# Causal attention in front of two feed-forward layers: the last rows of q and k are prepared beside q, and the turned tiles of a pair move one place

## The chip, the cores and the metric

One core of one Trainium2 chip runs the whole program. The metric is the device time of one execution in microseconds (us), the median of several.

## The reference

Attention runs over 4 batches of 8 heads, 576 positions of 64 elements. A query of block i (64 positions) sees the keys of the blocks up to i. The result, written as 2304 rows of 512, goes through a dense feed-forward layer (512 to 2048 to 512, ELU) and then a layer with 8 experts, of which each row uses at most one. The change touches only the attention:

```
scores = scale * np.matmul(q, k.transpose(0, 1, 3, 2))
scores = np.where(block_i >= block_j, scores, -1e9)
scores = scores - np.max(scores, axis=-1, keepdims=True)
attn = np.exp(scores)
attn = attn / (np.sum(attn, axis=-1, keepdims=True) + 1e-09)
return np.matmul(attn, v)
```

## The kernel before

Attention works on 16 pairs of heads. The two heads of a pair lie side by side on the partitions, 64 each. The 576 positions are four full tiles of 128 and one of 64, tile 4 (`LAST`), in which both heads share the 128 partitions. Every engine runs its own program, written as `step(kk, i)`, once for each pair n = 2*kk + i and twice more to drain. Steps 0 and 1 and the last four are unrolled; between them a loop holds two steps. Semaphores with counted values order the engines. Nothing is scheduled by a compiler: the order of the lines is the order of each engine's work.

In the step of pair n (`now`) five things lie side by side:

- **Scores of n.** TensorE multiplies q by k, tile after tile (`scores(n, i, u)`, L498 on), into the four banks of `s_ps`. Tiles 1 to 4 use three products of high and low halves of float32, so `scores(n, i, 0)` waits until the halves of this pair's q and k are there (`split_lo`). VectorE takes the row maximum (`row_max`, L332 and L335), ScalarE the exponential with its row sum (`exp`, L455).
- **Turning the probabilities.** TensorE transposes them through `t_ps`, a PSUM tensor of just two banks (`turn_pair` for tiles 0 and 1, `turn_head` for tiles 2 and 3, `turn_last` for tile 4, all by L533), and VectorE copies them to `pt` (L343, L351, L357, L364). The tiles 3 and 4 of pair n-1 (`past`) are turned in the step of n. The transposed reciprocals of the row sums and the last corner of tile 4 travel with tile 0 of n: `turned_corner` (L364) copies the corner and then the reciprocals to `r_rows` (L369).
- **Preparing pair n+1 (`after`).** TensorE transposes the raw q and k through the same two banks of `t_ps` (`prep`, L492): part 0 is q's four tiles, part 1 k's four tiles, part 2 the last 64 rows of both (`raw_tail`). ScalarE copies each part to `qk_f` (`prep_copy`: L436, L438, and L441 with L443). GpSimd then splits `qk_f` into halves in two pieces (`split`, L293 and L296): q's columns once part 0 is there, all the rest, k and the last rows, once all three parts are there (`prep_out` at 3n+3). After that it splits a slice of the next layer's weights (`wi_halves`, L304 and L309).
- **Values of n-1 and n-2.** TensorE multiplies v by `pt` into `o_ps` (`values`, L591), in a first part for `past` and a second part for `older` (n-2).
- **Final product of n-2.** VectorE multiplies `o_ps` by the reciprocals (`final`, L380). They have made a trip through memory for it: `r_rows` is stored (`store_recips`, L218) and loaded again, spread over the partitions, by four DMAs (`load_recips`, L224 and L227).

All DMAs are issued by SyncE, in one order per step: `load_v(n)`, `store(n-2)`, `store_recips(n-1)`, `load_qk(n+3)`, `load_recips(n-1)`, `load_wi(n+1)`. So the six DMAs of `load_qk` (up to the step of pair 12, the last that has any) stand between the store of the reciprocals and their load. `final` of a pair waits for its four loads (`r_in`), one step later.

Of the kernel before, what the change touches and what calls it, by code (L numbers as in the profile page):

```python
# [53 lines left out]
def attention(nc, q, k, v, attn_t, w_in, wi, x_raw, x_in):  # L54
# [27 lines left out]
    with ExitStack() as ctx:  # L82
# [243 lines left out]
        def _(dve):  # L326
# [11 lines left out]
            def turned_pair(n, i, u):  # L338

                wait(dve, pt_done, turns(n, u))  # L340
                c = u + 1
                bank = 1 - u
                dve.tensor_copy(pt[i][:, :, 0:c, u * P:(u + 1) * P],  # L343
                                t_ps[:, bank, 0:2 * c * P].rearrange("p (h j w) -> p h j w", h=2, w=P))\
                   .then_inc(turned, 1)
# [15 lines left out]
            def turned_corner(n, i, last):  # L361
# [3 lines left out]
                                      t_ps[0:TAIL, 1, 2 * P:3 * P].rearrange("p (h w) -> p h w", h=2))  # L365
# [3 lines left out]
                dve.tensor_copy(r_rows[:, :], t_ps[0:COLS, 1, R0:R0 + P]).then_inc(r_row_done, 1)  # L369
# [28 lines left out]
            def step(kk, i):  # L398
# [16 lines left out]
                if now:  # L415
                    turned_pair(*now, 0)
                    row_max(now[0], 3)
# [8 lines left out]
        def _(act):  # L426
            def prep_copy(n, i, g, bank):
# [9 lines left out]
                elif g == 1:  # L437
# [47 lines left out]
        def _(pe):  # L485
            def prep(n, i, g, bank):
# [3 lines left out]
                tiles = [raw[i][:, g, t] for t in range(FULL)] if g < 2 else [raw_tail[i]]  # L490
# [44 lines left out]
            def turn_pair(n, u, ahead=None, past=None):  # L535

                c = u + 1
                bank = 1 - u
                wait(pe, exp_done, exps(n, u, 1))
                if u == 0:  # L540
                    wait(pe, turned, turns(n - 1, LAST))
                    wait(pe, rec_done, n)
                elif ahead:
                    wait(pe, prep_out, 3 * ahead[0] + 2)
                else:
                    wait(pe, turned, turns(n - 1, 3, 0))
                for h in range(2):
                    for j in range(c):
                        last = turn(bank, (h * c + j) * P, prob[u][h][:, j * P:(j + 1) * P])
                if u == 0 and past:  # L550
                    turn(bank, 2 * P, prob4[:, FULL * P:S])
                    last = turn(bank, R0, recip[:, :])
                last.then_inc(pt_done, 1)

            def turn_head(n, u, h, ahead=None):

                wait(pe, exp_done, exps(n, u, h))
                if u == 3:
                    wait(pe, turned, turns(n, 2, h))
                elif h == 0:  # L560
                    wait(pe, turned, turns(n, 1))
                elif ahead:
                    wait(pe, prep_out, 3 * ahead[0] + 3)
                else:
                    wait(pe, turned, turns(n, 0))
# [11 lines left out]
            def turn_corner(n):  # L577

                wait(pe, turned, turns(n, LAST))
                wait(pe, rec_done, n + 1)  # L580
                turn(1, 2 * P, prob4[:, FULL * P:S])
                turn(1, R0, recip[:, :]).then_inc(pt_done, 1)

            def values(n, i, part):
                if part == 0:
                    wait(pe, turned, turns(n + 1, 0))
# [17 lines left out]
            def step(kk, i):  # L604
# [12 lines left out]
                if past:  # L617
                    turn_last(past[0])
                if now:
                    scores(*now, 2)  # L620
                    if after:
                        wait(pe, prep_out, 3 * after[0] + 1)
                        prep(*after, 1, 0)
                    turn_pair(now[0], 0, past=past)
                    scores(*now, 3)
                    turn_pair(now[0], 1, after)
                    if after:
                        wait(pe, turned, turns(now[0], 0))
                        prep(*after, 2, 1)
# [1195 lines left out]
```

## Time and profile before

| | |
|---|---|
| Median of 3 executions | 883.6 us (881.44 to 883.68) |
| The profiled execution | 883.7 us, of it 882.0 us span |
| TensorE busy (matmul) | 807.8 us, 92% of the span |
| VectorE, ScalarE, GpSimd busy | 538.2, 337.5, 241.4 us |
| Mean granted TensorE clock | 0.974 of full speed |
| Attention, from the first instruction to the last `final` | about 249 us |

The span is the time from the first to the last instruction of the core. "S" below is the moment at which TensorE begins the scores of a pair (L520), and "+3.4" means 3.4 us behind the S of that step. Idle time that the profile gives in brackets is that just before an instruction, with the operation that ended it.

### The profile page before, as it was taken

The page shows a single profiled execution, that of the slowest core. Times are in us where ns is not written, and L with a number is a line of the kernel's source. Part 1 is how long each engine was busy: PE and PEld are TensorE (multiplying, and loading weights), DVE is VectorE, ACT ScalarE, POOL GpSimd, SP SyncE. Part 2 cuts the span into 40 slices and gives each one's busy share as a digit, 9 for nine tenths or more (in the row PEclk, how much of TensorE's full clock was granted, in tenths as well). Part 3 has the DMA queues.
Part 4 walks back from the last instruction along what each step waited for, and adds up shares of the span by engine and source line. Part 5 has one row for each costly group of instructions (what it writes and reads, how often), then busy time and mean ns, then how long its engine had stood idle before and what let it go on. Part 6 is the DMA issues. An engine that isn't in the chain of part 4 may idle for free.

```text
span 882.0 us, 14734 instructions
## 1 busy us (share of the span) xinstructions
PE 807.8 (92%) x4618; PEld 672.2 (76%) x4619; DVE 538.2 (61%) x1318; ACT 337.5 (38%) x815; POOL 241.4 (27%) x232
## 2 busy tenths in 40 slices
PE   5787877888769999999999999999998899999995
PEld 4565655656559888888889888889886677887884
DVE  3565766666643337856866866863575699465342
ACT  3444545454323332222223223222345277354241
POOL 1545465455334411201201100210011222321221
PEclk9889999899989999999999999999999899999998
DMA  5344445453242431202002101013142389545100
GB/s 121 84 113 120 130 121 136 112 158 103 80 146 62 136 96 57 67 6 84 19 1 81 28 1 72 25 53 138 48 128 103 113 298 348 195 152 185 40 25 8
DMA packets 102913, 88.10 MB, mean 100 GB/s; under 512 B 66676, under 2 KB 78340, under 8 KB 102736
## 3 DMA queue, kind: packets, MB, share of 16 engines
q1 hardware_dynamic: 99808, 82.48, 30.2%
q0 software_dynamic: 3056, 5.00, 1.7%
q8 instruction: 26, 0.43, 0.2%
q14 instruction: 23, 0.19, 0.1%
HBM read 72.26 MB, written 18.34 MB: 103 GB/s over the span
## 4 chain that ended last, share of the span: by engine, by line
PE 66%; DVE 2%; issue 1%; DVEq 1%; ACT 0%; POOL 0%; POOLq 0%; ACTq 0%
PE h_ps L1570 11%; PE out_ps L1570 11%; PE h_ps L1571 11%; PE h_ps L1572 10%; PE out_ps L1572 10%; PE out_ps L1571 10%; PE out_ps L1705 1%; PE tr_ps L1670 1%; PE lg_ps L1621 1%; DVEq L871 0%; DVE xt_lo L1278 0%; DVE ht_lo L1317 0%; PE tr_ps L1610 0%; DVE x2t L1307 0%; DVE tile_ids L1287 0%
## 5 line engine op out<-in xcount | busy, mean ns | idle before, releaser
L1408 ACT ACTIVATE ex<-h_ps 128x384 f32<-128x384 f32 x96 | 47.2, 492 | 275.8 <-PE h_ps L1572 275.8
L1570 PE MATMUL h_ps<-xt_hi,wi_hi 128*128 128x384 f32 x384 | 132.3, 344 | 8.2 <-DVE xt_lo L1278 8.2
L1571 PE MATMUL h_ps<-xt_lo,wi_hi 128*128 128x384 f32 x384 | 130.3, 339 | 0.0
L1572 PE MATMUL h_ps<-xt_hi,wi_lo 128*128 128x384 f32 x384 | 130.3, 339 | 0.0
L1246 DVE TENSOR_SCALAR ex<-ex 128x384 f32<-128x384 f32 x96 | 35.1, 365 | 143.2 <-ACT ex L1408 142.1
L1570 PE MATMUL out_ps<-wo_hi,gt 128*128 128x512 f32 x288 | 114.6, 398 | 0.0
L1572 PE MATMUL out_ps<-wo_hi,gt 128*128 128x512 f32 x288 | 113.9, 396 | 0.0
L1571 PE MATMUL out_ps<-wo_lo,gt 128*128 128x512 f32 x288 | 113.3, 393 | 0.0
L455 ACT ACTIVATE prob<-s_ps,negmax 128x128 f32<-128x128 f32 (+2 forms) x144 | 77.7, 548 | 92.0 <-DVE negmax L332 92.0
L332 DVE TENSOR_REDUCE negmax<-s_ps 128x2 f32<-128x256 f32 (+1 forms) x64 | 51.3, 823 | 52.0 <-PE s_ps L528 49.0
L1128 DVE CUSTOM_DVE_ANT_0 x2t<-x,w_raw 128x512 bf16<-128x512 f32 x108 | 82.8, 807 | 0.4
L1570 PEld LDWEIGHTS h_ps<-xt_hi,wi_hi 128*128 128x128 f32 x384 | 72.5, 189 | 12.2 <-DVE xt_lo L1278 8.8
L1571 PEld LDWEIGHTS h_ps<-xt_lo,wi_hi 128*128 128x128 f32 x384 | 72.6, 189 | 3.1
L1572 PEld LDWEIGHTS h_ps<-xt_hi,wi_lo 128*128 128x128 f32 x384 | 72.5, 189 | 0.0
L1034 POOL DMA_INDIRECT route_table<-entry,slot x18 | 20.9, 1163 | 177.2 <-DVE slot L1207 161.0
L533 PE MATMUL t_ps<-ident,prob 128*128 128x128 f32 (+1 forms) x400 | 66.1, 300 | 2.6 <-DVE pt L357 0.9
L1026 POOL TENSOR_TENSOR xt_lo<-x_raw,xt_hi 128x384 fp32r<-128x384 f32 x20 | 28.4, 1419 | 142.6 <-ACT xt_hi L1422 142.4
L293 POOL TENSOR_TENSOR qk_hi<-qk_f,one 128x512 fp32r<-128x512 f32 (+1 forms) x30 | 36.0, 1200 | 106.2 <-ACT qk_f L436 54.5
L1572 PEld LDWEIGHTS out_ps<-wo_hi,gt 128*128 128x128 f32 x288 | 54.1, 188 | 13.4
L1570 PEld LDWEIGHTS out_ps<-wo_hi,gt 128*128 128x128 f32 x288 | 54.1, 188 | 9.4 <-DVE gt L1239 0.8
L1571 PEld LDWEIGHTS out_ps<-wo_lo,gt 128*128 128x128 f32 x288 | 54.1, 188 | 8.9
L533 PEld LDWEIGHTS t_ps<-ident,prob 128*128 128x128 f32 (+1 forms) x400 | 48.1, 151 | 12.5 <-issue 6.7
(174 smaller groups left out, 1661.7 us busy)
## 6 DMA issues: line engine op xcount, KB each, us to landing
w_raw<-in_moe_w_dram SPq DMA_DIRECT2D x56, 512.0 KB, 5.2
attn_t<-attn_sb SPq DMA_DIRECT2D x16, 288.0 KB, 2.1
x_raw<-attn_t SPq DMA_DIRECT2D x24, 192.0 KB, 2.5
out_dram<-x SPq DMA_DIRECT2D x18, 256.0 KB, 2.1
x_rows<-x SPq DMA_DIRECT2D x18, 256.0 KB, 2.5
raw_qk<-in_q_dram SPq DMA_DIRECT2D x32, 128.0 KB, 2.3
raw_qk<-in_k_dram SPq DMA_DIRECT2D x32, 128.0 KB, 2.4
v<-in_v_dram SPq DMA_DIRECT2D x32, 128.0 KB, 2.5
```

The costliest lines, as they stand in the source:

```text
L293: pool.tensor_tensor(qk_hi[i][:, a:b], qk_f[i][:, a:b], one[:, :].to_broadcast([P, b - a]), ALU.mult).then_inc(split_hi, 1)
L332: dve.tensor_reduce(heads_cols(negmax, u), s_pair(u), AX_X, ALU.max, negate=True).then_inc(max_done, 1)
L455: act.activation(dst, src, ACT.Exp, bias=negmax[:, c:c + 1], accum_out=rowsum[i][:, c:c + 1]).then_inc(exp_done, 1)
L533: return pe.transpose(t_ps[0:src.shape[1], bank, at:at + P], src, ident[:, :])
L1026: pool.tensor_tensor(xtk(b % 2, 1, k), x_raw[k][:, :], xtk(b % 2, 0, k).bitcast(F32), ALU.subtract).then_inc(x_lo_done, 1)
L1034: pool.indirect_dma_start(table, bass.IndirectOffsetOnAxis(ap=slot[j][:, 0:1], axis=0), entry[j][:, :], None, bounds_check=E * N - 1, oob_ ...
L1128: ins = dve.tensor_tensor_reduce(dot_rows[:, ((E + 1) * t + e) % 2], x2[s][:, :], all_skip if e == E else all_gates[:, e, :], 1.0, 0.0, AL ...
L1246: dve.tensor_scalar(e, e, 1.0, -1.0, ALU.min, ALU.add).then_inc(em_done, 1)
L1408: act.activation(ex[:, f % 2], h_ps[:, f % 2, 0:NB], ACT.Exp).then_inc(ex_done, 1)
L1570: pe.matmul(dst, stat[0], mov[0], start=start, stop=False, skip_group_check=True)
L1571: pe.matmul(dst, stat[0], mov[1], start=False, stop=False, skip_group_check=True)
L1572: return pe.matmul(dst, stat[1], mov[0], start=False, stop=stop, skip_group_check=True)
```

## The change

Five edits, all in the attention, which belong together because the two banks of `t_ps` change hands in another order:

1. The order of the preparation becomes q, last rows, k. The last rows are now part 1: TensorE transposes them right behind q, into bank 1, and ScalarE copies them right behind q. k is part 2, in bank 0, transposed behind the scores of tile 2 and copied ahead of the exponentials of tile 2.
2. `turn_last` (tile 4 of the past pair) moves from ahead of the scores of tile 2 to behind k's transposes. It now waits for ScalarE's copy of the last rows.
3. `turn_pair` for tile 0, with the corner and the reciprocals, moves behind the scores of tile 3 and from bank 1 to bank 0; tile 1 changes to bank 1 and waits for VectorE's copy of tile 4.
4. VectorE follows: reciprocals, `final`, maximum of tile 2, copy of tile 4, maximum of tile 3, corner and `r_rows`, tile 0, tile 1, maximum of tile 4.
5. `values` of the first part waits for the copy of tile 4, of the second part for that of the next pair's tile 0.

The cut diff:

```diff
@@ def step(kk, i), VectorE
                 if past:
                     for h in range(2):
                         turned_head(*past, 3, h)
+                if past:
+                    recips(past[0])
                 if older:
                     final(*older)
+                if now:
+                    row_max(now[0], 2)
                 if past:
-                    recips(past[0])
                     turned_last(*past)
                 if now:
-                    row_max(now[0], 2)
+                    row_max(now[0], 3)
                 if past:
                     turned_corner(*past, last=not now)
                 if now:
                     turned_pair(*now, 0)
-                    row_max(now[0], 3)
                     turned_pair(*now, 1)
@@ def step(kk, i), ScalarE
                     if after:
                         prep_copy(*after, 0, 0)
-                        prep_copy(*after, 1, 0)
+                        prep_copy(*after, 1, 1)
+                        prep_copy(*after, 2, 0)
                     exp(*now, 2)
                     exp(*now, 3)
-                    if after:
-                        prep_copy(*after, 2, 1)
                     exp(*now, LAST)
@@ def prep, TensorE
-                tiles = [raw[i][:, g, t] for t in range(FULL)] if g < 2 else [raw_tail[i]]
+                tiles = [raw_tail[i]] if g == 1 else [raw[i][:, g // 2, t] for t in range(FULL)]
@@ def turn_last
-            def turn_last(n):
+            def turn_last(n, ahead):
                 wait(pe, exp_done, exps(n, LAST, 0))
-                wait(pe, turned, turns(n, 3, 1))
+                wait(pe, *((prep_out, 3 * ahead[0] + 2) if ahead else (turned, turns(n, 3, 1))))
@@ def step(kk, i), TensorE
                 if after:
                     wait(pe, turned, turns(past[0], 3, 0)) if past else pe.wait_ge(prep_out, 3)
                     prep(*after, 0, 0)
-                if past:
-                    turn_last(past[0])
+                    wait(pe, turned, turns(past[0], 3, 1)) if past else pe.wait_ge(prep_out, 3)
+                    prep(*after, 1, 1)
                 if now:
                     scores(*now, 2)
-                    if after:
-                        wait(pe, prep_out, 3 * after[0] + 1)
-                        prep(*after, 1, 0)
-                    turn_pair(now[0], 0, past=past)
+                if after:
+                    wait(pe, prep_out, 3 * after[0] + 1)
+                    prep(*after, 2, 0)
+                if past:
+                    turn_last(past[0], after)
+                if now:
                     scores(*now, 3)
-                    turn_pair(now[0], 1, after)
-                    if after:
-                        wait(pe, turned, turns(now[0], 0))
-                        prep(*after, 2, 1)
+                    turn_pair(now[0], 0, after, past)
+                    turn_pair(now[0], 1)
                     scores(*now, LAST)
```

No instruction is added or taken away on ScalarE, VectorE, GpSimd or SyncE, and no DMA changes; what moves shows in each engine's order.

ScalarE, one step (here step 0, which is unrolled): before, the first L436 and L438 are the copies of q and k, L441 and L443 those of the last rows, L455 the exponentials by width.

```order
L436 ACTIVATE qk_f<-t_ps 128x512
L438 ACTIVATE qk_f<-t_ps 128x512
L455 ACTIVATE prob_0,rowsum<-s_ps,negmax 128x384
L455 ACTIVATE prob_1,rowsum<-s_ps,negmax 128x384
L455 ACTIVATE prob_0,rowsum<-s_ps,negmax 128x512
L455 ACTIVATE prob_1,rowsum<-s_ps,negmax 128x512
L441 ACTIVATE qk_f<-t_ps 64x64 x2
L443 ACTIVATE qk_f<-t_ps 128x64
L455 ACTIVATE prob,rowsum<-s_ps,negmax 128x576
```

ScalarE, the same step after the change (the lines are numbered one higher):

```order
L437 ACTIVATE qk_f<-t_ps 128x512
L442 ACTIVATE qk_f<-t_ps 64x64 x2
L444 ACTIVATE qk_f<-t_ps 128x64
L439 ACTIVATE qk_f<-t_ps 128x512
L456 ACTIVATE prob_0,rowsum<-s_ps,negmax 128x384
L456 ACTIVATE prob_1,rowsum<-s_ps,negmax 128x384
L456 ACTIVATE prob_0,rowsum<-s_ps,negmax 128x512
L456 ACTIVATE prob_1,rowsum<-s_ps,negmax 128x512
L456 ACTIVATE prob,rowsum<-s_ps,negmax 128x576
```

The copy that completes `prep_out` is now k's, ahead of four exponentials; before it was that of the last rows, behind them.

VectorE, one step of the loop before, from `final` to the maximum of tile 4 (L335); L332 are the maxima of tiles 2 and 3, L357 is tile 4, L364 and L369 the corner and `r_rows`, L343 tiles 0 and 1:

```order
L380 TENSOR_TENSOR attn_sb<-o_ps,r_sb 128x576
...
L374 RECIPROCAL recip<-guarded 128x9
...
L357 COPY pt<-t_ps 128x4x2x64
...
L332 TENSOR_REDUCE negmax<-s_ps 128x2
...
L364 COPY pt<-t_ps 64x2x64
...
L369 COPY r_rows<-t_ps 9x128
...
L343 COPY pt<-t_ps 128x2x128
...
L332 TENSOR_REDUCE negmax<-s_ps 128x2
...
L343 COPY pt<-t_ps 128x2x2x128
...
L335 TENSOR_REDUCE negmax<-s_ps 128x1
```

VectorE, the same place after the change:

```order
L373 RECIPROCAL recip<-guarded 128x9
...
L379 TENSOR_TENSOR attn_sb<-o_ps,r_sb 128x576
...
L332 TENSOR_REDUCE negmax<-s_ps 128x2
...
L356 COPY pt<-t_ps 128x4x2x64
...
L332 TENSOR_REDUCE negmax<-s_ps 128x2
...
L363 COPY pt<-t_ps 64x2x64
...
L368 COPY r_rows<-t_ps 9x128
...
L342 COPY pt<-t_ps 128x2x128
...
L342 COPY pt<-t_ps 128x2x2x128
...
L335 TENSOR_REDUCE negmax<-s_ps 128x1
```

The copy to `r_rows` now stands behind the maximum of tile 3.

## Rows read from the trace of the kernel before

**Rows 1.** Stretches: from:to, length, each engine's busy time, granted clock, DMA share, GB/s.

```profile
55.10:71.50 16.40, 13.95 (x99) 10.31 (x99) 9.25 (x16) 6.96 (x24) 7.64 (x7) 0.81 0.43 112
86.60:167.80 81.20, 66.51 (x596) 49.51 (x596) 53.76 (x96) 41.43 (x144) 45.81 (x37) 1.00 0.48 129
```

**Rows 2.** Waits in the attention: engine, line, released by: us in total, times, longest.

```profile
PE s_ps L520 <- POOL qk_lo L296: 37.0, 15, 2.7
```

**Rows 3.** Timeline, TensorE, one step of the loop: start, us, engine, line, operation [idle before].

```profile
100.10 0.49 PE L520 MATMUL s_ps<-qk_f 64*128 64x128 f32 x4 [2.44 <-POOL qk_lo L296]
...
113.63 0.49 PE L520 MATMUL s_ps<-qk_f 64*128 64x128 f32 x4 [2.45 <-POOL qk_lo L296]
```

**Rows 4.** Timeline, ScalarE and GpSimd, the same step.

```profile
105.67 0.60 ACT L438 ACTIVATE qk_f<-t_ps 128x512 f32<-128x512 f32 x1 [1.11 <-PE t_ps L492]
105.83 1.28 POOL L296 TENSOR_TENSOR qk_lo<-qk_f,qk_hi 128x512 fp32r<-128x512 f32 x1
...
109.72 0.43 ACT L441 ACTIVATE qk_f<-t_ps 64x64 f32<-64x64 f32 x2
...
110.47 1.36 POOL L293 TENSOR_TENSOR qk_hi<-qk_f,one 128x704 fp32r<-128x704 f32 x1 [3.36 <-ACT qk_f L443]
...
111.91 1.66 POOL L296 TENSOR_TENSOR qk_lo<-qk_f,qk_hi 128x704 fp32r<-128x704 f32 x1
```

**Rows 5.** Timeline, VectorE, the same step.

```profile
103.53 0.76 DVE L380 TENSOR_TENSOR attn_sb<-o_ps,r_sb 128x576 f32<-128x576 f32 x1 [0.18 <-issue]
...
104.33 0.67 DVE L357 COPY pt<-t_ps 128x512 f32<-128x512 f32 x1
105.08 0.96 DVE L332 TENSOR_REDUCE negmax<-s_ps 128x2 f32<-128x768 f32 x1
106.10 0.28 DVE L364 COPY pt<-t_ps 64x128 f32<-64x128 f32 x1
106.31 0.27 DVE L369 COPY r_rows<-t_ps 9x128 f32<-9x128 f32 x1
...
107.05 1.23 DVE L332 TENSOR_REDUCE negmax<-s_ps 128x2 f32<-128x1024 f32 x1
```

**Rows 6.** Timeline, SyncE's DMA issues, the same step and the next.

```profile
106.64 0.31 SPq L218 DMA_DIRECT2D recip_rows<-r_rows  x1
107.91 0.97 SPq L195 DMA_DIRECT2D raw_qk<-in_q_dram  x2
...
111.83 0.50 SPq L224 DMA_DIRECT2D r_sb<-recip_rows  x1
...
118.10 0.66 SPq L197 DMA_DIRECT2D v<-in_v_dram  x1
119.22 0.37 SPq L211 DMA_DIRECT2D attn_t<-attn_sb  x1
```

**Rows 7.** Timeline, the last pair: its reciprocals are stored, loaded and used.

```profile
242.36 0.29 SPq L218 DMA_DIRECT2D recip_rows<-r_rows  x1
243.59 0.45 SPq L224 DMA_DIRECT2D r_sb<-recip_rows  x1
...
248.12 0.76 DVE L380 TENSOR_TENSOR attn_sb<-o_ps,r_sb 128x576 f32<-128x576 f32 x1 [5.78 <-issue]
```

**Rows 8.** Timeline: S of pair 1, `final` of pairs 0 and 11, S of pair 15.

```profile
26.02 0.49 PE L520 MATMUL s_ps<-qk_f 64*128 64x128 f32 x4 [2.66 <-POOL qk_lo L296]
...
45.04 0.76 DVE L380 TENSOR_TENSOR attn_sb<-o_ps,r_sb 128x576 f32<-128x576 f32 x1 [1.42 <-PE o_ps L591]
...
202.65 0.76 DVE L380 TENSOR_TENSOR attn_sb<-o_ps,r_sb 128x576 f32<-128x576 f32 x1 [0.18 <-issue]
...
226.39 0.49 PE L520 MATMUL s_ps<-qk_f 64*128 64x128 f32 x4 [2.48 <-POOL qk_lo L296]
```

**Rows 9.** DMA issues in the attention: transfer, count, KB each, median us to landing.

```profile
x_raw<-attn_t SPq DMA_DIRECT2D x4, 192.0 KB, 3.7
...
r_sb<-recip_rows SPq DMA_DIRECT2D x30, 16.0 KB, 2.5
```

More of the change, by code:

```diff
@@ L341, in turned_pair @@
                 c = u + 1
-                bank = 1 - u
                 dve.tensor_copy(pt[i][:, :, 0:c, u * P:(u + 1) * P],
-                                t_ps[:, bank, 0:2 * c * P].rearrange("p (h j w) -> p h j w", h=2, w=P))\
+                                t_ps[:, u, 0:2 * c * P].rearrange("p (h j w) -> p h j w", h=2, w=P))\
                    .then_inc(turned, 1)
@@ L364, in turned_corner @@
                 ins = dve.tensor_copy(pt[i][0:TAIL, :, FULL, FULL * P:S],
-                                      t_ps[0:TAIL, 1, 2 * P:3 * P].rearrange("p (h w) -> p h w", h=2))
+                                      t_ps[0:TAIL, 0, 2 * P:3 * P].rearrange("p (h w) -> p h w", h=2))
                 if last:
@@ L368, in turned_corner @@
                 wait(dve, r_stored, 16 * n)
-                dve.tensor_copy(r_rows[:, :], t_ps[0:COLS, 1, R0:R0 + P]).then_inc(r_row_done, 1)
+                dve.tensor_copy(r_rows[:, :], t_ps[0:COLS, 0, R0:R0 + P]).then_inc(r_row_done, 1)
             def recips(n):
@@ L436, in prep_copy @@
                     act.activation(qk_f[i][:, Q:K], src[:, :], ACT.Copy, scale=SCALE).then_inc(prep_out, 1)
-                elif g == 1:
+                elif g == 2:
                     act.activation(qk_f[i][:, K:K + FULL * P], src[:, :], ACT.Copy).then_inc(prep_out, 1)
@@ L537, in turn_pair, with turn_head @@
                 c = u + 1
-                bank = 1 - u
                 wait(pe, exp_done, exps(n, u, 1))
-                if u == 0:
+                if u:
                     wait(pe, turned, turns(n - 1, LAST))
+                else:
+                    if ahead:
+                        wait(pe, prep_out, 3 * ahead[0] + 3)
+                    else:
+                        wait(pe, turned, turns(n - 1, 3, 0))
                     wait(pe, rec_done, n)
[L543 to L546, printed above, removed]
                 for h in range(2):
                     for j in range(c):
-                        last = turn(bank, (h * c + j) * P, prob[u][h][:, j * P:(j + 1) * P])
+                        last = turn(u, (h * c + j) * P, prob[u][h][:, j * P:(j + 1) * P])
                 if u == 0 and past:
-                    turn(bank, 2 * P, prob4[:, FULL * P:S])
-                    last = turn(bank, R0, recip[:, :])
+                    turn(0, 2 * P, prob4[:, FULL * P:S])
+                    last = turn(0, R0, recip[:, :])
                 last.then_inc(pt_done, 1)
-            def turn_head(n, u, h, ahead=None):
+            def turn_head(n, u, h):
                 wait(pe, exp_done, exps(n, u, h))
[L558 to L565, printed above, removed]
+                wait(pe, turned, turns(n, 2, h) if u == 3 else turns(n, h))
                 for j in range(u + 1):
@@ L577, in turn_corner @@
             def turn_corner(n):
-                wait(pe, turned, turns(n, LAST))
+                wait(pe, turned, turns(n, 3, 0))
                 wait(pe, rec_done, n + 1)
-                turn(1, 2 * P, prob4[:, FULL * P:S])
-                turn(1, R0, recip[:, :]).then_inc(pt_done, 1)
+                turn(0, 2 * P, prob4[:, FULL * P:S])
+                turn(0, R0, recip[:, :]).then_inc(pt_done, 1)
             def values(n, i, part):
+                wait(pe, turned, turns(n + 1, 0) if part else turns(n, LAST))
                 if part == 0:
-                    wait(pe, turned, turns(n + 1, 0))
                     wait(pe, v_in[i], 48 * (n // 2) + 48)
@@ L636, in step @@
                     for h in range(2):
-                        turn_head(now[0], 2, h, after)
+                        turn_head(now[0], 2, h)
             all_pairs(step)(pe)
```

## The prediction

> **What bounds the kernel now.** I read the attention alone: the two feed-forward layers are untouched and begin when it ends, so what it saves or loses, the whole saves or loses. First the busy time by stretch. In the six undisturbed steps TensorE is busy 66.5 of 81.2 us, the most of any engine, yet not all of it; in the stretch from 55.1 to 71.5 the granted clock averages 0.81 and one step takes 16.4 us where others take 13.5 [rows 1]. Then the waits: before the scores of a pair TensorE stands still for GpSimd's split, 15 times, 37.0 us in all [rows 2]. Then one step in order of time. From S to S it takes 113.63 - 100.10 = 13.53 us; at the end of it TensorE, which has then turned tile 2, idles 2.45 us [rows 3]. So **TensorE's own work is 13.53 - 2.45 = 11.08 us** a step. The chain behind the idle time: ScalarE copies the last rows only behind the exponentials of tile 3 (109.72); with that copy GpSimd can begin its second piece at 110.47, 3.36 us idle, and ends it at 111.91 + 1.66 = 113.57; the scores follow at 113.63 [rows 3, 4].
>
> **Edit 1, preparation.** k's copy completes the three parts. ScalarE has 1.11 us of idle time ahead of that copy now [rows 4]; the copy of the last rows (0.67 us with its gaps, 109.72 to 110.39) falls into it, so k's copy stays where it was within some 0.2 us and ends at +6.2. GpSimd is then still busy with the first piece, which ends at 105.83 + 1.28 = 107.11, +7.0 [rows 4]. The second piece takes 113.57 - 110.47 = 3.1 us and ends at about +10.2 in place of +13.47: 3.3 us earlier, 0.9 us ahead of TensorE's 11.08. **The wait of 2.45 us goes.** If only this counted, a step would last 11.1 us. In step 0 TensorE has no past tiles to turn, the split remains last and S of pair 1 gains the whole 3.3, less 0.3 for k's transposes and copy, which in the opening wait for q's copy: 26.02 [rows 8] becomes 23.0.
>
> **Edits 2, 3 and 5, TensorE.** The same transposes in another order, so no busy time. `turn_last` waits for the last rows' copy, done at about +5.2, when TensorE gets there at +5.1; the scores of tile 3 begin near +5.9, as now. Tile 1 waits for VectorE's copy of tile 4. While VectorE is on time that is hidden by the scores of tile 3; what holds VectorE back is the next point.
>
> **Edit 4, VectorE: what is late next.** `r_rows` is now copied behind the maximum of tile 3. Behind it hangs a ring that closes through `final`: `final` of one pair, then on the same engine the copy of `r_rows` for the next pair, then SyncE stores it, issues the six DMAs of `load_qk`, issues the four loads of the reciprocals, they land, and the next `final` may run. What stands behind `final` on VectorE (the maximum of tile 2, so ScalarE's exponentials and in the end TensorE) goes round with it. Link by link:
>
> - `final` to the end of the `r_rows` copy: now 103.53 to 106.58, 3.05 us. After the change, the durations of `final`, maximum of tile 2, copy of tile 4, maximum of tile 3, corner, `r_rows` are 0.76 + 0.96 + 0.67 + 1.23 + 0.28 + 0.27 = 4.17; back to back, each begins some 0.08 before the one ahead has ended (L364 ends at 106.38, L369 begins at 106.31), five times 0.08 off: **3.77** [rows 5].
> - To the store's issue 0.06 [rows 5, 6]. The store issue takes 0.31. Between it and `load_qk` SyncE works out addresses and tests a wait. Now 107.91 - 106.95 = 0.96 us lie there, but TensorE's transposes of the last rows end only in that gap. The bounds are 0 and 0.96; I take 0.46, the gap between 118.76 and 119.22 of a store whose wait was long fulfilled, the nearest row [rows 6]. Sum **0.83**.
> - `load_qk` to the first load of reciprocals: 111.83 - 107.91 = **3.92** [rows 6].
> - From the issue of the first of the four loads to a `final` that waits for nothing else: 248.12 - 243.59 = **4.53** [rows 7].
>
> The ring is 3.77 + 0.83 + 3.92 + 4.53 = **13.1 us**. Today it is 0.7 to 0.8 shorter on VectorE and not last: the loads begun at 111.83 could release a `final` at 116.36, while `final` comes at S + 3.43 = 117.06 [rows 3, 5, 6]. The change takes 2.45 us from one chain and makes the other, hidden by 0.7 us now, the bound: a step goes from 13.53 to 13.1 where both groups of DMAs are issued, and TensorE idles near 2 us in it, in the middle. Edit 3's wait of tile 1 for tile 4's copy shows there.
>
> **The low clock.** From the first `final` to that of pair 11, eleven steps take 202.65 - 45.04 = 157.6 us, 14.33 each [rows 8], 0.8 more than 13.53: the price of steps like the one at 0.81. TensorE then does its work 2.9 us slower (16.4 against 13.5) in the worst of them [rows 1]. In the ring of 13.1 TensorE has 2 us to spare, and its pauses get shorter and more than one; I charge the low clock 0.5 us in all in the opening, and nothing in the ring.
>
> **The sum**, in times of `final`:
>
> - First `final`. In the step of pair 1 `turn_last` starts with the last rows' copy (+5.1), the scores of tile 3 end 1.5 later (+6.6), the maximum takes 1.15 and the two copies 0.5: the copy of `r_rows` ends at +8.2. Then 9.3 of the ring, and 0.5 for the clock: 23.0 + 8.2 + 9.3 + 0.5 = 41.0, against 45.04: **4.0 saved**.
> - Eleven rings of 13.1: 144.1 against 157.6: **13.5 saved**.
> - From `final` of pair 11 on no `load_qk` is issued. The ring falls to 3.8 + 0.1 + 1.23 (243.59 - 242.36, the store must land) + 4.53 = 9.6 [rows 7], below 11.08: TensorE bounds. S of pair 14 follows 6.6 behind `final` 11 (behind it: maximum of tile 2, two exponentials, scores and values), one step of 11.1, and from S of pair 15 to the end 20.9, where it was 248.12 - 226.39 = 21.7: I take 0.8 off, since the corner no longer waits for the copy of tile 4. 38.6 against 45.5: **6.9 saved**.
>
> 24.4 us in all. The profiled execution took 883.7 us, 0.1 above the median of 883.6, so the sum needs no correction: **859.3, say 859 us**.
>
> **Rivals.**
>
> - *The ring, with slower transfers.* For it: in the ring, `load_wi` and `load_v` are issued right behind the loads of the reciprocals, and loads in the same stage took 3.7 us to land where these take 2.5 [rows 9]. With 1.2 more the ring is 14.3: eleven times 1.2 is 13 us, 872; with the gap of 0.96 too, 878. Against it: the DMA engines are busy 0.48 of the time [rows 1], and the order of issue is the same.
>   "DMA: Bandwidth & Descriptors" of the Trainium skill (Latency and other measured facts) gives HBM access 0.2 us on average and 2 us at high load and calls it the largest part of a transfer's fixed cost; by that the landing could grow by up to 1.8 us, an estimate from the page, and the whole would come to 879. No row here shows these loads slowed.
> - *No ring: TensorE alone bounds.* It needs an early landing or a ring below 11.1, so 2 us less than my links. Then S of pair 1 at 23.0, first `final` at 23.0 + 11.1 + 3.4 = 37.5, eleven steps of 11.06 to 159.2, 36.5 to the end: 195.7, so 831 us. For it: TensorE is the busiest engine [rows 1]. "Perfetto Trace Analysis" of the Trainium skill (Identifying the Most-Contended Engine) says to improve that engine first; the wait removed is TensorE's own. Against it: every link of the ring but one gap is a row. Between the two, the ring with a gap of 0 is 12.7 and gives 854.
> - *Slower than before, by the clock.* In the step from 55.1 on TensorE ran partly at the lower of its two levels (1.2 for 2.4 GHz); the mean of 0.81 cost 2.9 us [rows 1], so 2.9 for 0.19 x 16.4 = 3.1 us of lost clock, 0.93 each. If the new pauses, one or two in each step, keep the clock down, TensorE's 11.08 grow and bound the step. To be slower than now the eleven steps must take 13.1 + (24.4 + 2.7) / 11 = 15.6 each; TensorE alone takes so long from a loss of (15.6 - 11.08) / 0.93 = 4.9 us a step, a granted clock below 0.69 in every step. At 0.6 the step is 17.6 and the whole 859 + 11 x 4.5 = 909. Against it: the pauses get shorter.
> - *It gives nothing.* The ring would have to be 13.1 + 24.4 / 11 = 15.3, 2.2 us above the sum of its rows. No row shows that.
>
> **How the numbers follow.** The ring near 13.1 (853 to 866) gets 0.62; the ring with slower transfers (866 to 880) 0.18; a shorter ring or none (831 to 853) 0.13; nothing won 0.04; slower by the clock 0.03. The time is that of the first. The range takes it whole and the larger part of its neighbours: 848 to 873. A change of 0.3%, 2.7 us, is what a measurement of this kernel can tell from none; faster 0.93, same 0.04, slower 0.03.
>
> **What would show it.** TensorE's wait for the split (37.0 us) gone or below 5. `final` with idle time of about 3 us before it, at equal distances of 13.1, in steps 3 to 13. New waits of TensorE before tile 1 (for L356) and of ScalarE before the exponentials of tile 2. SyncE's store of the reciprocals about 3.8 us behind each `final`, `load_qk` 0.8 behind that. Steps of 11.1 at the very end. Wrong, if `final` comes 3.4 us behind S without a wait, if the distances are not 13.1, or if the granted clock of the attention is below now's.

## The result

| | before | after |
|---|---|---|
| Median | 883.1 us (881.44 to 883.68, 4 runs) | 855.6 us (854.28 to 859.39, 4 runs) |
| Ratio, 95% interval | | 0.970 (0.966 to 0.973) |
| Profiled execution, its span | 883.7, 882.0 | 859.4, 857.7 |
| Last `final` | 248.12 | 220.69 |
| From the last `final` to the end of the span | 633.9 | 637.0 |

Faster by 3.0%, 27.5 us. The profiled execution is the slowest of the four; the times of the trace below are to be held against its 859.4, not against the median.

The waits of after, in the attention (the columns of [rows 2]). GpSimd's split no longer stands in TensorE's list; the row of [rows 2] has no successor. In its place VectorE waits 12 times for the reciprocals before `final`, and TensorE for the copy of tile 4:

```profile
ACT prob L456 <- DVE negmax L332: 74.3, 44, 4.4
...
DVE attn_sb L379 <- DMA r_sb<-recip_rows: 33.4, 12, 3.5
...
PE t_ps L533 <- DVE pt L356: 14.4, 11, 1.9
```

One turn of the ring, from `final` to `final`. First VectorE's timeline of after, the successor of [rows 5], then SyncE's issues, the successor of [rows 6]:

```profile
105.03 0.76 DVE L379 TENSOR_TENSOR attn_sb<-o_ps,r_sb 128x576 f32<-128x576 f32 x1 [2.81 <-DMA r_sb<-recip_rows]
105.71 0.95 DVE L332 TENSOR_REDUCE negmax<-s_ps 128x2 f32<-128x768 f32 x1
106.57 0.68 DVE L356 COPY pt<-t_ps 128x512 f32<-128x512 f32 x1
107.17 1.22 DVE L332 TENSOR_REDUCE negmax<-s_ps 128x2 f32<-128x1024 f32 x1
108.30 0.27 DVE L363 COPY pt<-t_ps 64x128 f32<-64x128 f32 x1
108.50 0.27 DVE L368 COPY r_rows<-t_ps 9x128 f32<-9x128 f32 x1
...
118.22 0.76 DVE L379 TENSOR_TENSOR attn_sb<-o_ps,r_sb 128x576 f32<-128x576 f32 x1 [3.12 <-DMA r_sb<-recip_rows]
```

```profile
108.79 0.31 SPq L218 DMA_DIRECT2D recip_rows<-r_rows  x1
109.42 0.97 SPq L195 DMA_DIRECT2D raw_qk<-in_q_dram  x2
...
113.31 0.51 SPq L224 DMA_DIRECT2D r_sb<-recip_rows  x1
...
115.14 0.60 SPq L227 DMA_DIRECT2D r_sb<-recip_rows  x1
```

The links are 3.74 us on VectorE (105.03 to 108.77), 0.65 to `load_qk`, 3.89 to the first load, 4.91 to the next `final`: 13.19. From the first `final` to that of pair 11, the timeline gives (the successors of [rows 8]):

```profile
22.10 0.38 PE L520 MATMUL s_ps<-qk_f 64*128 64x128 f32 x2
...
30.05 0.27 DVE L368 COPY r_rows<-t_ps 9x128 f32<-9x128 f32 x1
...
39.15 0.76 DVE L379 TENSOR_TENSOR attn_sb<-o_ps,r_sb 128x576 f32<-128x576 f32 x1 [2.68 <-DMA r_sb<-recip_rows]
...
182.29 0.76 DVE L379 TENSOR_TENSOR attn_sb<-o_ps,r_sb 128x576 f32<-128x576 f32 x1 [2.17 <-DMA r_sb<-recip_rows]
...
220.69 0.76 DVE L379 TENSOR_TENSOR attn_sb<-o_ps,r_sb 128x576 f32<-128x576 f32 x1 [5.55 <-issue]
```

(182.29 - 39.15) / 11 = **13.01 us** a turn on average, and 38.40 from `final` 11 to the last. The single distances run from 12.24 to 13.56. Then the stretches, columns as in [rows 1]. Of after: the eleven turns, a stretch in them at the low level of the clock (the only one), and the first 10 us of TensorE's work in the feed-forward layer:

```profile
39.20:182.30 143.10, 128.30 (x1089) 90.89 (x1085) 95.55 (x177) 78.09 (x264) 83.33 (x66) 0.99 0.52 139
122.40:125.80 3.40, 3.40 (x17) 1.62 (x17) 1.15 (x2) 1.78 (x6) 1.68 (x2) 0.54 0.39 89
...
225.39:235.39 10.00, 9.46 (x30) 8.87 (x31) 4.99 (x10) 2.65 (x6) 3.43 (x4) 0.53 0.73 234
```

Of before, the same eleven distances, one of the six low stretches in its attention, and the same 10 us of the feed-forward layer:

```profile
45.00:202.60 157.60, 130.69 (x1092) 97.31 (x1090) 99.51 (x176) 75.81 (x263) 83.98 (x66) 0.94 0.47 125
...
54.60:61.40 6.80, 6.28 (x37) 4.86 (x38) 2.66 (x5) 1.72 (x8) 2.75 (x3) 0.50 0.31 86
...
252.82:262.82 10.00, 9.46 (x42) 8.36 (x43) 6.59 (x13) 4.34 (x9) 5.03 (x5) 0.84 0.76 236
```

So the 14.5 us won in the eleven distances (157.6 - 143.1) are of two kinds. The undisturbed step fell from 13.53 to 13.01, which is 5.7 us; the other 8.8 are steps of before that lasted longer than 13.53 because TensorE ran at 1.2 GHz in part of them. After has one such stretch, and the distances around it stay 13.03 and 13.05: the slower TensorE is covered by the ring. Ahead of the first `final`, which comes at 39.15 for 45.04, before also has two low stretches and after none. At the start of the feed-forward layer it is the other way round: 0.53 against 0.84 of full speed over 10 us is 3.1 us of full clock lost, and after needs 3.1 us more from the last `final` to the end. Whether the one causes the other is taken up under the last experiment.

### The profile page after: what moved, and what is told of

The parts are those of the page before. It is cut to its first block, busy times and chain, and to the rows that moved or that the text cites. A ratio compares the mean times of both kernels' runs of the same rounds, so it can differ in the third digit from the quotient of the medians.

```text
span 857.7 us, 14746 instructions
## 1 busy us (share of the span) xinstructions
PE 804.7 (94%) x4618; PEld 665.6 (78%) x4619; DVE 531.8 (62%) x1318; ACT 340.1 (40%) x815; POOL 241.4 (28%) x232
## 4 chain that ended last, share of the span: by engine, by line
PE 69%; DVE 2%; issue 1%; DVEq 1%; ACT 0%; POOL 0%; POOLq 0%; ACTq 0%
PE h_ps L1563 11%; PE out_ps L1563 11%; PE h_ps L1564 11%; PE h_ps L1565 11%; PE out_ps L1565 11%; PE out_ps L1564 11%; PE out_ps L1698 1%; PE tr_ps L1663 1%; PE lg_ps L1614 1%; DVEq L864 0%; DVE xt_lo L1271 0%; PE tr_ps L1603 0%; DVE ht_lo L1310 0%; DVE x2t L1300 0%; DVE tile_ids L1280 0%
## 5 line engine op out<-in xcount | busy, mean ns | idle before, releaser
L533 PE MATMUL t_ps<-ident,prob 128*128 128x128 f32 (+1 forms) x400 | 61.0, 284 | 15.1 <-DVE pt L356 14.4
L1027 POOL DMA_INDIRECT route_table<-entry,slot x18 | 20.9, 1164 | 177.2 <-DVE slot L1200 161.0
L533 PEld LDWEIGHTS t_ps<-ident,prob 128*128 128x128 f32 (+1 forms) x400 | 42.2, 140 | 29.7 <-DVE pt L356 17.6
L332 DVE TENSOR_REDUCE negmax<-s_ps 128x2 f32<-128x256 f32 (+1 forms) x64 | 51.1, 819 | 11.7 <-PE s_ps L528 11.5
```

The lines of the kernel that those rows point to most:

```text
L332: dve.tensor_reduce(heads_cols(negmax, u), s_pair(u), AX_X, ALU.max, negate=True).then_inc(max_done, 1)
L533: return pe.transpose(t_ps[0:src.shape[1], bank, at:at + P], src, ident[:, :])
L1027: pool.indirect_dma_start(table, bass.IndirectOffsetOnAxis(ap=slot[j][:, 0:1], axis=0), entry[j][:, :], None, bounds_check=E * N - 1, oob_ ...
```

## The experiments

All ratios are against the kernel before, measured beside each group of runs (medians 882.5, 882.5, 884.1 and 884.4 us), with their 95% interval; "distance" is the mean of the eleven distances from `final` to `final`, unless said otherwise. Kernels with added transposes (the fillers, four of them) do extra work on TensorE whose results nobody uses.

### Is it the ring? Loads of the reciprocals moved in SyncE's order

`load_qk`'s 3.9 us stand in the ring only because of the order of issue. The same edit was made in after and in before:

```diff
@@ step, SyncE
                     store_recips(past[0])
-                if (ahead := pair(kk, i, 3)):
-                    load_qk(*ahead)
                 if past:
                     load_recips(past[0])
+                if (ahead := pair(kk, i, 3)):
+                    load_qk(*ahead)
```

In after:

> The changed kernel with one edit on SyncE: the four loads of the reciprocals are issued ahead of the six DMAs of load_qk. Ring theory (final, r_rows, store, load_qk, loads of the reciprocals, final bounds the step at 13.0 us): 3.9 us of issue leave the ring and 1.2 of waiting for the store to land come in, so the ring falls to about 9.7 and TensorE's own 11.1 bounds; distances of final 13.0 -> 11.1 to 11.4 (SyncE's own issue time per step comes near 11.3), 12 x 1.8 = about 21 us less than the changed kernel: 832 to 838 us. Rival A (a step of 13 us is bound by something else, GpSimd or ScalarE or the transfers themselves): within 2 us of 855.6. Rival B (the loads land later when load_qk follows right behind, contention): between, 840 to 850.

853.2 us, 0.967 (0.963 to 0.970): hardly apart from the change's own 0.970. The distance fell to (175.35 - 37.25) / 11 = 12.55, not to the expected 11.1 to 11.4; without the last turn (14.23 us, in which SyncE also issues four loads for the next layer, L31) it is 12.39. In before:

> The same edit on SyncE in the kernel before. Ring theory: the ring is hidden there by 0.7 us behind the wait for GpSimd's split, so the edit gives nothing: within 1.5 us of 883.1, the wait of 2.45 us before each scores still there, steps of 13.5. Rival (the place of the reciprocals' loads mattered before as well, the change only shifted it): 5 us faster or more.

883.4 us, 1.001 (0.999 to 1.003), as expected: in before the ring is hidden. The miss in after shows in SyncE's own queue. Its timeline in the first of the two:

```profile
105.87 0.35 SPq L218 DMA_DIRECT2D recip_rows<-r_rows  x1
107.71 0.49 SPq L224 DMA_DIRECT2D r_sb<-recip_rows  x1
...
109.52 0.60 SPq L227 DMA_DIRECT2D r_sb<-recip_rows  x1
110.43 0.99 SPq L195 DMA_DIRECT2D raw_qk<-in_q_dram  x2
...
116.63 0.65 SPq L197 DMA_DIRECT2D v<-in_v_dram  x1
117.86 0.37 SPq L211 DMA_DIRECT2D attn_t<-attn_sb  x1
118.34 0.31 SPq L218 DMA_DIRECT2D recip_rows<-r_rows  x1
```

The loads must wait until the store has landed, and now nothing is issued meanwhile: 1.84 us from 105.87 to 107.71. From there on SyncE waits for nothing until the next store, 12.47 us behind the first. The `r_rows` of that store had been ready since 116.13, 2.2 us before the issue at 118.34; in after the issue follows 0.02 us behind `r_rows`. SyncE itself has become the bound.

### One more DMA in the ring

```diff
@@ step, SyncE
-                if past:
-                    load_recips(past[0])
                 if (after := pair(kk, i, 1)):
                     load_wi(after[0])
+                if past:
+                    load_recips(past[0])
```

> The changed kernel with load_wi (one DMA, about 0.65 us of issue) moved from behind the loads of the reciprocals to ahead of them. Ring theory: each us put into the ring costs a us in each of the 12 steps that have a load_qk, and hardly any after: distances of final 13.0 -> 13.7, 12 x 0.65 = 8 us more than 855.6, 862 to 865 us; if load_wi has to wait for GpSimd's wi_lo there, more. Rival (SyncE has slack, the step is bound by engines): 855.6 within 2.

867.9 us, 0.983 (0.979 to 0.987), 3 us above the expected range. The issue takes 0.60 us with its gap, the distance grew by 0.50, to 13.51: (188.28 - 39.67) / 11. From the store to the first load of the reciprocals it takes 5.15 to 5.18 us in most turns, where after takes 4.51 to 4.55: 0.6 more. From there to `final` it takes 4.56 on average for 4.68: 0.1 less. SyncE's timeline:

```profile
116.42 0.46 SPq L232 DMA_DIRECT2D wi_raw<-in_moe_w_in_dram  x1
117.02 0.49 SPq L224 DMA_DIRECT2D r_sb<-recip_rows  x1
```

The whole lost more than the eleven turns explain: from `final` 11 to the last it takes 42.0 us for 38.4. `load_wi` is also issued in the last steps, where no `load_qk` stands ahead of it, and there it has to wait for GpSimd, 5.7 us in two times, with the loads of the reciprocals behind it (SyncE's waits from 186 to 230: releaser, us in total, times, longest):

```profile
SPq L232 <- POOL wi_lo L309: 5.7, 2, 4.0
```

The expectation had named this wait, but not where it would come.

### A shorter link on VectorE

```diff
@@ step, VectorE
                     turned_last(*past)
-                if now:
-                    row_max(now[0], 3)
                 if past:
                     turned_corner(*past, last=not now)
                 if now:
+                    row_max(now[0], 3)
```

> The changed kernel with one edit on VectorE: turned_corner (corner and r_rows) ahead of the maximum of tile 3. Ring theory: 1.15 us leave the ring's VectorE link, distances of final 13.0 -> 11.9, 11 x 1.15 = 13 us less: 841 to 846 us, although the maximum of tile 3 and with it ScalarE's exponentials come 0.5 us later against final. Rival (the maximum of tile 3 and the exponentials behind it bound): no gain or a loss, 855 to 862.

**843.8 us, 0.956 (0.952 to 0.960)**, as expected. VectorE's timeline:

```profile
99.51 0.76 DVE L379 TENSOR_TENSOR attn_sb<-o_ps,r_sb 128x576 f32<-128x576 f32 x1 [1.74 <-DMA r_sb<-recip_rows]
...
101.89 0.27 DVE L368 COPY r_rows<-t_ps 9x128 f32<-9x128 f32 x1
102.09 1.20 DVE L332 TENSOR_REDUCE negmax<-s_ps 128x2 f32<-128x1024 f32 x1
```

The link is 102.16 - 99.51 = 2.65 us for 3.74, and the distances are (170.73 - 38.77) / 11 = 12.0 for 13.0. Lengthening one link by 0.6 us and shortening another by 1.1 moved the step by 0.5 and by 1.0, each the way and nearly the size of the link: the ring is shown, from both sides.

### SyncE full, or the ring? Both edits together, and a better cut

First both: the loads of the reciprocals ahead of `load_qk`, and the corner ahead of the maximum of tile 3.

> The edits of e1 and e4 together in the changed kernel. In e1 the steps came out at 12.4 and not 11.1. Theory S (SyncE itself is full there: its 16 issues and the 1.2 to 1.8 us in which it stands waiting for the store to land make 12.4 us a step): e4's shorter VectorE link gives nothing on top, distances of final 12.3 to 12.4, 850 to 854 us, slower than e4 alone (843.8). Theory R (in e1 it is still a ring through VectorE): 1.15 less than 12.4, so 11.3, 838 to 842.

851.7 us, 0.964 (0.959 to 0.969), distance (175.93 - 36.84) / 11 = 12.64 (12.46 without the last turn): slower than the corner alone. The 1.1 us taken off VectorE bring nothing where SyncE bounds. Then the corner ahead of the maximum as before, and `load_qk` cut in two, so that q's three DMAs fill the time in which the store lands, and k's three stand behind the loads:

```diff
@@ step, SyncE
                     store_recips(past[0])
                 if (ahead := pair(kk, i, 3)):
                     load_qk(*ahead)
                 if past:
                     load_recips(past[0])
+                if ahead:
+                    load_k(*ahead)
@@ load_qk
                 load(q, n, raw[i][:, 0], raw_tail[i][0:TAIL], qk_in[i])
+
+            def load_k(n, i):
                 load(k, n, raw[i][:, 1], raw_tail[i][TAIL:P], qk_in[i])
@@ ahead of the steps
             load_qk(0, 0)
+            load_k(0, 0)
...
```

> The changed kernel with e4's edit, and load_qk cut in two on SyncE: q's three DMAs ahead of the loads of the reciprocals, so that SyncE is issuing while the store lands, k's three behind them. Theory S: SyncE's step is 12.4 - 1.2 = 11.2, the ring is 12.0 - 1.95 = 10.1, TensorE's own work 11.1: distances of final 11.2 to 11.5, 0.5 to 0.8 less in each of 12 steps than e4: 834 to 839 us, the fastest of all. Rival (transfers slowed by closer spacing): no better than 843.8.

**836.7 us, 0.948 (0.943 to 0.952)**: 5.2% under before and 2.2% under the change. The distance is (161.31 - 37.10) / 11 = 11.29. SyncE's timeline and the stretch between the two `final`s:

```profile
96.99 0.31 SPq L220 DMA_DIRECT2D recip_rows<-r_rows  x1
97.63 0.97 SPq L195 DMA_DIRECT2D raw_qk<-in_q_dram  x2
...
99.57 0.52 SPq L226 DMA_DIRECT2D r_sb<-recip_rows  x1
...
102.11 1.07 SPq L195 DMA_DIRECT2D raw_qk<-in_k_dram  x2
```

```profile
37.10:161.30 124.20, 124.20 (x1108) 92.21 (x1106) 97.75 (x176) 79.50 (x271) 84.75 (x67) 1.00 0.61 161
```

TensorE is busy in the whole stretch, at full clock, and waits for nothing in it. Now it is TensorE that bounds the step; from this a further cut of the ring should bring nothing, which no run tried.

### What the clock took in before

TensorE's pause of before [rows 3] was filled with 16 transposes of a constant, without any other edit:

```diff
@@ scores, TensorE
                 if u == 0:
                     wait(pe, exp_done, exps(n - 1, 3, 1))
+                    for c in range(FILL):
+                        pe.transpose(s_ps[:, (c % 2) * BANK:(c % 2) * BANK + P], ident[:, :], ident[:, :])
                     wait(pe, split_lo, 2 * n + 2)
```

> The kernel before, and TensorE does 16 transposes of a constant (2.0 us) into score columns that are overwritten right after, in its pause of 2.45 us ahead of each pair's scores; the wait for GpSimd's split stays. Question: how much of the 27 us comes from the granted clock. Theory (the six low stretches in the attention of before follow these pauses and cost what the steps there are longer than 13.53, some 10 us): the granted clock stays at 1.00 through the attention, every step 13.5, 871 to 875 us. Rival (the low stretches cost nothing, or the wait alone explains the gain): 881 to 885.

871.3 us, 0.986 (0.982 to 0.991), as expected. The waits and the stretch of that kernel:

```profile
PE s_ps L523 <- POOL qk_lo L297: 10.5, 15, 0.8
```

```profile
20.00:235.00 215.00, 198.95 (x1767) 153.31 (x1766) 138.52 (x249) 104.35 (x364) 114.67 (x90) 1.00 0.46 120
```

The first distance is 13.24, the others 13.53 to 13.55, and the granted clock is 1.00: 11 of the 27 us come from the clock alone, without the split's wait being moved at all. In the profiled executions 3.5 of them lie ahead of the first `final` (41.59 for 45.04) and 8.9 in the eleven distances (148.7 for 157.6). In before the clock had fallen in 6 stretches of the attention, in or just behind pauses of 2.4 to 2.7 us of TensorE.

### One edit undone: k's copy back behind the exponentials

```diff
@@ step, ScalarE
                         prep_copy(*after, 1, 1)
-                        prep_copy(*after, 2, 0)
                     exp(*now, 2)
                     exp(*now, 3)
+                    if after:
+                        prep_copy(*after, 2, 0)
```

> The changed kernel with k's copy on ScalarE put back behind the exponentials of tile 3, where the last rows' copy was. Ring theory: tile 0's turn, the corner and r_rows wait for that copy, so 2.5 to 2.8 us enter the ring between final and r_rows: distances of final 15.5 to 15.8, 885 to 892 us, and TensorE still does not wait for GpSimd's split. Rival (the early copy matters through GpSimd's split): the wait for the split of about 2 us a step returns, steps of 13.5, 870 to 875.

921.6 us, 1.043 (1.038 to 1.048): the direction was right, the size far off. The distance is (234.19 - 46.95) / 11 = 17.0, and the granted clock is 0.80 from 48 to 208, with a low stretch of 6.8 us in every step. Two causes were left: the clock (C), or the late copy itself (W). The first try filled the new pause with 20 transposes:

> e6 came out at 921.6 us, 30 above what I expected of it: steps of 17.1, with a stretch of 6.8 us at the lower clock in each of them behind TensorE's pause of 3.4 us ahead of tile 0's turn. Here e6 with 20 transposes of a constant (2.5 us at the full clock) in that pause, into score columns that are overwritten later. Theory C (the clock adds to the ring: TensorE's slowed work keeps it from being ahead of final, so the links from final to r_rows grow): clock 1.00, distances of final 15.6 to 16.0, 885 to 895 us. Rival W (the ring in e6 is 17.1 by its waits alone, the clock is a bystander): distances stay at 17, 912 us or more.

918.4 us, 1.037 (1.034 to 1.041), distance (233.34 - 45.66) / 11 = 17.1, and it decided nothing: the 20 transposes took 4.07 us, and the turning of tile 0 began 1.5 us behind the end of k's copy, so they held it up themselves. The second try had 10:

```diff
@@ turn_pair, TensorE
                 else:
+                    wait(pe, exp_done, exps(n, 2, 1))
+                    for _ in range(10):
+                        pe.transpose(s_last()[:, 0:P], ident[:, :], ident[:, :])
                     if ahead:
                         wait(pe, prep_out, 3 * ahead[0] + 3)
```

> The change with k's copy put back behind the exp of tile 3, as in the run that took 921.6, and 10 transposes of a constant on TensorE in its pause, half of the 20 that themselves held tile 0's turn; what they write is not used. The 20 took 4.07 us, so 10 take about 2.0 us and end before k's copy does (119.06 minus 116.68 was 2.4 us). Theory C, the clock adds to the ring: without k's low stretches the step falls from 17.1 towards the ring that k's copy lengthens, 13.0 plus 2.5 to 3 = 15.5 to 16.0, so finals 15.5 to 16.0 us apart and 885 to 898 us. Theory W, the late copy alone makes the 17 us (work that waits behind it on ScalarE and VectorE, not the clock): finals stay 16.8 to 17.3 apart and the time is 912 us or more, whatever the granted clock shows. Between the two (898 to 912) each has a part.

908.5 us, 1.028 (1.024 to 1.031), between the two. The distance is (224.19 - 45.67) / 11 = 16.2, the granted clock 0.91. The timeline shows what the ring goes through now, VectorE and ScalarE of this kernel:

```profile
111.25 0.76 DVE L379 TENSOR_TENSOR attn_sb<-o_ps,r_sb 128x576 f32<-128x576 f32 x1 [2.39 <-DMA r_sb<-recip_rows]
111.92 0.95 DVE L332 TENSOR_REDUCE negmax<-s_ps 128x2 f32<-128x768 f32 x1
...
112.98 0.58 ACT L456 ACTIVATE prob<-s_ps,negmax 128x384 f32<-128x384 f32 x1 [2.48 <-DVE negmax L332]
...
116.05 0.59 ACT L439 ACTIVATE qk_f<-t_ps 128x512 f32<-128x512 f32 x1
...
117.85 0.27 DVE L368 COPY r_rows<-t_ps 9x128 f32<-9x128 f32 x1
```

`final`, the maximum of tile 2, four exponentials, k's copy (done at 116.64), the turning of tile 0 and with it of the reciprocals, `r_rows` (done at 118.12): 6.87 us where after takes 3.74. That is 3.1 us more in the ring, 13.0 + 3.1 = 16.1, near the measured 16.2. In the kernel without filler the same link takes 7.99 in the turn shown:

```profile
97.94 0.76 DVE L379 TENSOR_TENSOR attn_sb<-o_ps,r_sb 128x576 f32<-128x576 f32 x1 [0.30 <-DMA r_sb<-recip_rows]
98.92 0.96 DVE L332 TENSOR_REDUCE negmax<-s_ps 128x2 f32<-128x768 f32 x1 [0.22 <-PE s_ps L529]
...
105.66 0.27 DVE L368 COPY r_rows<-t_ps 9x128 f32<-9x128 f32 x1
```

There even the maximum of tile 2 waits for TensorE's scores. Averaged over the eleven turns the link takes 7.1 us with the 10 transposes and 7.8 without. So W has at most 3.2 us a step (16.23 - 13.01) and C at least 0.8 (17.02 - 16.23): 35 and 9 us in the eleven distances. The spans of the two profiled executions differ by 62.2 us (919.9 - 857.7); the other 18 lie at both ends, the first `final` 7.8 later, and 12.3 more from `final` 11 to the last, less 2 us behind it. There the chain through ScalarE bounds too: a step of 14.4 without `load_qk` in the kernel with 10 transposes, 224.19 to 238.58.

How much a wholly full clock would still give, since 0.09 of it was missing, can be estimated from the same trace. Four of its turns have no low stretch. Two of them, from 94.52 and 159.47, follow upon one of 6.8 us; TensorE is late in them, and the link takes 7.64 and 7.70. The other two, from 127.44 and 192.32, have it at 6.62 and last 15.89 and 15.75 us. The first of these:

```profile
127.44:143.33 15.89, 13.74 (x119) 10.31 (x121) 8.78 (x16) 7.29 (x26) 8.86 (x8) 1.00 0.42 106
```

With all steps near 15.8, W would have 2.8 us a step and C 1.2. That is an estimate from two turns; no run kept the clock full.

### The start of the feed-forward layer

The next kernel is the best one with 48 transposes behind TensorE's last work of the attention:

```diff
@@ TensorE, behind the steps
             all_pairs(step)(pe)
+            for c in range(48):
+                pe.transpose(s_ps[:, (c % 2) * BANK:(c % 2) * BANK + P], ident[:, :], ident[:, :])
```

> e8's kernel (836.7 us) with 48 transposes of a constant, 5.9 us, that TensorE does at the end of the attention, where it now stands still for some 8 us until the feed-forward begins. In the profiles of before the low stretch at the feed-forward's start was 6.8 us and from the last final to the end 633.9 us passed, in the changed kernel 13.7 us and 637.0, in e8 10.2 us and 635.4. Theory (the low stretch, not the transfers, makes that difference of 3 us, and the pause makes the low stretch): the low stretch gone or 3.4 us, from the last final to the end 630 to 632 us, the whole 832 to 834. Rival (the start of the feed-forward is set by VectorE's splits and the transfers): 635 and 836.7 as before.

836.4 us, 0.946 (0.942 to 0.949): no gain. The stretches from the last `final` on, first of the kernel with `load_qk` cut, then of this one:

```profile
199.19:203.89 4.70, 0.00 (x0) 0.00 (x0) 1.99 (x7) 0.00 (x0) 1.30 (x9) 0.50 0.27 71
203.89:213.89 10.00, 9.92 (x40) 9.40 (x41) 5.32 (x12) 4.05 (x9) 5.44 (x5) 0.73 0.78 234
```

```profile
198.81:203.51 4.70, 2.43 (x23) 2.19 (x21) 1.99 (x7) 0.00 (x0) 1.30 (x9) 1.00 0.18 69
203.51:213.51 10.00, 9.30 (x34) 8.10 (x35) 5.35 (x10) 3.02 (x6) 3.43 (x4) 0.66 0.78 235
```

The transposes lifted the clock of the pause from 0.50 to 1.00, and in the 10 us behind it the clock came down all the same, to 0.66 for 0.73. The low stretch was put off, not avoided. From the last `final` to the end of the span this kernel takes 635.8 us, the other 635.4. That the 3.1 us which after loses here are the clock's fits the rows (0.53 against before's 0.84), but no run made it go away, so it is argued and not shown. One run speaks against the whole of it: with the pauses filled, the kernel before had 0.69 in these 10 us, 1.5 us of full clock less than before's 0.84, and took only 0.5 us longer from the last `final` to the end (634.4 for 633.9).

## Why the prediction was right

It said 859 us, 848 to 873, faster by the ring. Measured: 855.6, and the ring is the mechanism.

- **Edit 1, the split.** The wait of 37.0 us [rows 2] is gone, as said. S of pair 1 was forecast at 23.0 and came at 22.10. GpSimd's second piece was forecast to end at +10.2, and in the step from S = 111.72 it ends at 121.82, +10.1.
- **Edit 4, the ring.** Forecast 3.77 + 0.83 + 3.92 + 4.53 = 13.1; measured 3.74 + 0.65 + 3.89 + 4.91 in the step shown, 13.01 on average. The link taken by choice, a gap of 0.46 behind the store, is 109.42 - 109.10 = 0.32. The loads took 4.45 to 5.04 us to `final`, 4.68 on average, for 4.53 in [rows 7]; the two, each 0.15, offset each other. That this sum of links, and not TensorE, sets the step is shown by the run with one more DMA (+0.50), the one with the corner first (-1.0) and the same edit in before (nothing).
- **Edits 2, 3 and 5.** TensorE's wait for the copy of tile 4 came as said, 14.4 us in 11 times, 1.3 each for "near 2"; TensorE was recorded busy 128.3 / 11 = 11.7 us a turn, not 11.1.
- **First `final`.** Forecast 41.0, measured 39.15, 1.9 earlier: S of pair 1 0.9, the rest of the first ring 8.83 (30.32 to 39.15) for 9.3, and the 0.5 charged for the clock in the opening, which was not lost. `r_rows` at +8.22 was met (+8.2).
- **Eleven rings.** Forecast 144.1, measured 143.1. The forecast had the distances equal; they were 12.24 to 13.56: from the store to the first load most turns take 4.5 us, the first two 4.85 and 5.23, the last 3.89.
- **The end.** Forecast 6.6 + 11.1 + 20.9 = 38.6, measured 6.69 + 11.08 + 20.63 = 38.40 (S of pairs 14 and 15 at 188.98 and 200.06).
- **The low clock.** Nothing was charged in the ring; one low stretch came and cost nothing there. What the prediction did not say is how much of the gain is the clock's: it took before's mean of 14.33 a step and so had it in the sum, but called the wait's removal the gain. The filled pause shows 11 us for the clock alone.
- **What was left out.** "What it saves or loses, the whole saves or loses" was not exact. The attention ended 3.0 us earlier than forecast (220.69 for 41.0 + 144.1 + 38.6 = 223.7), and the rest took 3.1 us longer than before. In the profiled execution the two errors cancel, by luck (859.4 for 859.3).

**The rivals.** *Slower transfers*: the loads to `final` took 4.68 us on average where the forecast had 4.53, so 0.15 of the 1.2 that this rival needed, and 0.5 in the worst turn. The Trainium skill, "DMA: Bandwidth & Descriptors" (Latency and other measured facts), allows 2 us for HBM at high load; with DMA engines busy 0.52 of the time no row here shows that. *No ring*: 831 was TensorE's own bound; the change did not reach it. The Trainium skill, "Perfetto Trace Analysis" (Identifying the Most-Contended Engine), says to improve the engine with the highest occupancy first, and would judge TensorE by the share of its peak arithmetic (MFU) and by the busy time of its weight loads rather than of its matmuls. In [rows 1] (the second and third of the busy times) the weight loads have 49.5 of 81.2 us, fewer than VectorE's 53.8, so it does not plainly name TensorE here. The trace agrees with the rule in half: TensorE's wait could be taken away, yet another 19 us came only from the order of work on VectorE and SyncE. With the ring cut to TensorE's length the kernel took 836.7, with a first `final` at 37.10 for the rival's 37.5 and distances of 11.29 on average for 11.06. *Slower by the clock*: not here, but one edit less and it is there: k's copy behind the exponentials gave 921.6, at a clock of 0.80.

## What to carry to other kernels

When a wait is removed, add up the closed chains that it hid, on every queue that they cross, SyncE's issues included; the longest one is the new step, and its links can be read in the trace of before. Then cut that chain at the cheapest link: here two short copies ahead of a maximum, and three DMAs issued while a store lands, were worth 19 us, more than half of what the whole reordering had brought. A pause of TensorE costs more than its length where the clock falls with it (11 us in the kernel before).

## What the runs showed of the hardware

- **The clock can fall at short pauses.** Pauses of 2.4 to 2.7 us, one in each step, led to stretches of 3.4 or 6.8 us at 1.2 GHz in 6 places of the attention of before; with the pauses filled there was one, of 3.4 us in the opening, and the kernel was 11 us faster. It did not fall in every step: six steps from 86.6 to 167.8 with the same pauses ran at 1.00 [rows 1].
- **Work just ahead did not keep it up.** With 23 of the 48 transposes recorded in the pause before the feed-forward layer, the pause showed 1.00, and the 10 us behind it 0.66.
- **SyncE can be full with 16 DMAs a step.** Each issue takes 0.3 to 0.7 us and they stand 0.5 to 1.2 apart. A step took 12.4 us where SyncE had one wait for a store to land and no other, and 11.29 where it filled that wait with three of its issues.
- **A ring can hide a slow engine.** In after a low stretch of 3.4 us at 0.54 left the distances at 13.03 and 13.05. With one more DMA in the ring there were six such stretches, and VectorE's link of the ring was 3.73 to 3.74 us in all eleven turns, as in after. With k's copy late it hid nothing: the same link was 6.62 us in two turns at full clock, and 7.8 on average with a low stretch in every turn.
